# Attention and Fourier mixing of the next batch interleaved with the first MLP of this one, split weights streamed from DRAM

## The chip, the cores and the metric

The kernel runs on one core of a Trainium2 chip. The metric is the device time of one execution in microseconds (us). Engines: PE is TensorE (PEld its weight loads), DVE is VectorE, ACT is ScalarE, POOL is GpSimd, SP is SyncE, which only issues DMAs here.

## The reference

Four batches (B = 4) of 768 tokens, 8 heads of 64, so a width of 512 (DM). Three parts in a row:

```
# windowed attention: per chunk of 32 queries, 8 memory keys and up to 56 neighbours
scores = scale * q_c @ [mem_k, k_ctx].T ;  a = softmax(scores) ;  x = a @ [mem_v, v_ctx]
# Fourier mixing, layer norm, first MLP (512 -> 2048 -> 512)
mixed = real(fft(fft(x, axis=1), axis=2)) ;  u = x + mixed
un = (u - mean) / sqrt(var + 1e-6)
y = u + maximum(un @ w_ch1, 0) @ w_ch2
# gated convolution (512 -> 1024 -> 512)
h = maximum(y @ w_in, 0) ;  conv_out = three taps along the sequence, per channel
out = (h * sigmoid(conv_out)) @ w_out
```

All of it is fp32 in and out.

## The kernel before

Matmuls that need precision are done as three products of fp32r halves: each operand is split into a rounded `_hi` part (a ScalarE copy) and the rest `_lo` (a VectorE or GpSimd subtraction), and `lo*hi + hi*lo + hi*hi` is summed in PSUM. Scores, values and all transposes are plain fp32.

Each engine has a program of its own, written out in order, with semaphores between them. There are three stages.

**Attention and Fourier mixing** (`attention_and_fourier`, line 144 on). A batch has six tiles of 128 tokens (TILES). Per tile: `scores` on TensorE (L490), shift by the maximum and normalisation on VectorE (`softmax`, L388 to L412, with ScalarE's exponential L293 between), `turn` (four transposes, L501) with ScalarE's copy to `p_blk` (L304), `values` (L514) and ScalarE's copy to `x_sb` (L317). Then the Fourier part: the six tiles of x are folded by symmetry (`fold`, L204 to L212; two pairs on GpSimd, one on VectorE), split, multiplied by tables along the sequence (`seq` 0 to 7, nine products each, L525) and along the width (`dim` 0 and 1, 27 products), combined and mirrored (L431 to L446) and transposed back (`mix` 0 to 5, L579). The table ORDER gives for each engine how steps of one batch stand between those of the batch before (a prime behind a step: one batch behind, two primes: two). The buffers of q and k have three tiles (NB), those of v six. x and the mixed tokens are stored to DRAM (`x_scratch`, `mix_scratch`).

**First MLP** (`channel_mlp`), in half batches of 384 tokens. It loads x and the mixed tokens, adds them, normalises, transposes (`turn`, L780) and splits them. All 16 blocks of 128 hidden channels (M1T = 16) of both weights are split once and stay in SBUF. A slot of TensorE is: `expand(m+1)` (twelve products of 384 columns, L791) and `contract(m)` (nine of 512 columns, L806) into three PSUM accumulators (BACC). ScalarE makes `h_hi` (L706), VectorE `h_lo` (L767). At the end of a half, VectorE adds the accumulators to u (L957). 8 halves of 16 slots are 128 slots; the first three expansions and the first two contractions stand at the end of the first stage.

**Gated convolution** (`gated_conv`), which loads y from DRAM (L1039), and the taps (L1049); its weights are loaded and split, and the first batch's y transposed, beside the last half of the MLP (`first_sync`, `first_scalar`, `first_vector`, `first_tensor`). Its first product is L1153.

SyncE's queue issues nearly all DMAs, in order, each behind its waits; the four Fourier tables come from GpSimd's queue.

Of the kernel before, what the change touches and what calls it, by code (L numbers as in the profile page):

```python
# [19 lines left out]
NB = 3  # L20
MIX = 3
# [10 lines left out]
M2T = FF2 // P  # L32
SCALE = float(D) ** -0.5
# [40 lines left out]
class Core:  # L74
# [3 lines left out]
    def __init__(self, nc, ctx, ident):  # L78
# [4 lines left out]
        self.st_x = [self.sem(f"st_x{i}") for i in range(2)]  # L83
        self.st_mix = [self.sem(f"st_mix{i}") for i in range(MIX)]
        self.scored, self.valued, self.x_ready = self.sem("scored"), self.sem("valued"), self.sem("x_ready")
        self.mix_turned, self.mix_ready = self.sem("mix_turned"), self.sem("mix_ready")
        self.st_y = [self.sem(f"st_y{i}") for i in range(2)]
        self.w_ready, self.acc_done, self.y_ready = self.sem("w_ready"), self.sem("acc_done"), self.sem("y_ready")
        self.block = ctx.enter_context(nc.Block())

    def sem(self, name):
# [3 lines left out]
ORDER = {  # L95
    "tensor": (
        "turn5' scores0 seq7'' values5' scores1 "
        "turn0 dim1'' mix0'' mix1'' mix2'' scores2 values0 turn1 seq0' mix3'' values1 seq1' "
        "mix4'' scores3 turn2 seq2' seq3' mix5'' values2 scores4 turn3 seq4' values3 "
        "dim0' scores5 turn4 seq5' values4 seq6'",  # L100
        "turn5' seq7'' values5' dim1'' mix0'' mix1'' mix2'' seq0' mix3'' seq1' mix4'' seq2' mix5'' seq3' mlp3 "
        "seq4' dim0' mlp5 seq5' seq6' mlp7",
        "seq7'' dim1'' mlp9 mix0'' mix1'' mlp10 mix2'' mix3'' mlp11 mix4'' mix5''",
    ),
    "scalar": (
# [13 lines left out]
        "seq6' mlp7",  # L119
        "seq7'' mlp8 dim1'' mlp9 mlp10",  # L120
    ),
}


def attention_steps(engine, attention, starts, ends):

    on = (attention, starts, ends)  # L130
    steps = []
# [1281 lines left out]
```

## Time and profile before

| | |
|---|---|
| timed runs | 1111.16, 1111.59, 1113.31 us; median 1111.59 |
| profiled execution, own time | 1113.53 us |
| its span in the trace | 1111.7 us |
| its mean granted TensorE clock | 0.972 |
| busy in the span | PE 1030.3 us, DVE 494.6, ACT 324.2, POOL 145.2 |
| DMA | 98.75 MB moved, mean 89 GB/s |

The span runs from the first to the last instruction in the trace; start and end of the program lie around it. Busy time of PE counts a matmul until its modelled end, so neighbouring matmuls overlap, and the time of one is read from start to start. The granted clock is given in parts of the upper of TensorE's two levels (1.2 and 2.4 GHz): 1.00 is the upper, 0.50 the lower.

### The profile page before, as it was taken

How to read it: one execution, taken by the hardware profiler on the slowest of the kernel's cores; microseconds unless marked ns; L12 is line 12 of the kernel's file. 1: busy time of each engine (PE TensorE's matmuls, PEld its weight loads, DVE VectorE, ACT ScalarE, POOL GpSimd, SP SyncE). 2: the span in 40 equal slices, each digit the busy share in tenths (PEclk: the TensorE clock that was granted, in tenths of full speed). 3: DMA queues.
4: the chain of work that ended last, by engine and by line, in shares of the span. 5: the costliest groups of instructions: out<-in, count | busy, mean ns of one | idle time of the engine just before them, and what ended most of it. 6: DMA issues, size and time to landing. Idle time of an engine off the chain costs nothing.

```text
span 1111.7 us, 15656 instructions
## 1 busy us (share of the span) xinstructions
PE 1030.3 (93%) x6348; PEld 930.2 (84%) x6348; DVE 494.6 (44%) x749; ACT 324.2 (29%) x551; POOL 145.2 (13%) x97
## 2 busy tenths in 40 slices
PE   5769686968899999999999999999999999999998
PEld 5658676957799989898989898989989798797996
DVE  4466566556453323323222232222439449185390
ACT  3334534445531111111111111111415324243242
POOL 0414141240000000000000000000003204023041
PEclk9889888969999999999999999999999999999999
DMA  9956556153522002020020200105201020110001
GB/s 370 366 190 216 190 193 226 57 170 123 180 86 85 1 1 85 1 85 1 1 85 0 85 0 28 57 1 143 96 29 57 32 83 1 57 57 28 29 1 57
DMA packets 53236, 98.75 MB, mean 89 GB/s; under 512 B 6464, under 2 KB 18880, under 8 KB 52928
## 3 DMA queue, kind: packets, MB, share of 16 engines
q1 hardware_dynamic: 49152, 88.17, 23.0%
q10 hardware_dynamic: 3456, 6.29, 1.5%
q0 software_dynamic: 576, 3.55, 0.8%
q8 instruction: 38, 0.62, 0.2%
q14 instruction: 14, 0.11, 0.0%
HBM read 72.84 MB, written 25.17 MB: 88 GB/s over the span
## 4 chain that ended last, share of the span: by engine, by line
PE 64%; issue 20%; DVE 6%; POOL 6%; DMA 3%; ACT 2%; SPq 0%; ACTq 0%; POOLq 0%; DVEq 0%
PE ps L806 24%; PE ps L791 24%; POOL g_lo L1219 6%; PE ps L525 5%; PE ps L490 3%; PE ps L514 3%; DMA k_nat<-in_k 2%; PE ps L1163 2%; PE ps L579 1%; PE ps L780 1%; PE ps L501 1%; DVE m_all L440 1%; DVE probs L412 1%; DMA y_scratch<-u_sb 0%; DVE stat L406 0%
## 5 line engine op out<-in xcount | busy, mean ns | idle before, releaser
L791 PE MATMUL ps<-un_hi,w 128*128 128x384 f32 x1024 | 284.4, 338 | 2.3 <-ACT mix_sb L350 2.3
L806 PE MATMUL ps<-w,h_hi 128*128 128x512 f32 x768 | 242.0, 396 | 0.0
L767 DVE SCALAR_TENSOR_TENSOR h_lo<-ps,h_hi 128x384 fp32r<-128x384 f32 x128 | 71.3, 557 | 278.7 <-ACT h_hi L706 278.7
L791 PEld LDWEIGHTS ps<-un_hi,w 128*128 128x128 f32 x1024 | 186.6, 188 | 6.7 <-ACT mix_sb L350 2.5
L706 ACT ACTIVATE h_hi<-ps 128x384 fp32r<-128x384 f32 x128 | 63.0, 492 | 374.9 <-PE ps L791 374.5
L791 PE MATMUL ps<-un_lo,w 128*128 128x384 f32 x512 | 171.6, 335 | 0.0
L806 PEld LDWEIGHTS ps<-w,h_hi 128*128 128x128 f32 x768 | 144.3, 188 | 28.3
L806 PE MATMUL ps<-w,h_lo 128*128 128x512 f32 x384 | 151.0, 393 | 0.9 <-DVE h_lo L767 0.9
L1153 PE MATMUL ps<-y_hi,v 128*128 128x384 f32 x512 | 130.6, 334 | 0.8 <-issue 0.8
L1163 PE MATMUL ps<-v,g_hi 128*128 128x512 f32 x384 | 120.5, 395 | 0.0
L1118 DVE SCALAR_TENSOR_TENSOR conv<-h_pad,taps,conv 128x768 f32<-128x768 f32 x64 | 100.4, 1568 | 2.3
L791 PEld LDWEIGHTS ps<-un_lo,w 128*128 128x128 f32 x512 | 96.2, 188 | 4.6
L1219 POOL TENSOR_TENSOR g_lo<-conv,g_hi 128x768 fp32r<-128x768 f32 x32 | 68.6, 2148 | 194.1 <-ACT g_hi L1087 194.1
L1153 PEld LDWEIGHTS ps<-y_hi,v 128*128 128x128 f32 x512 | 92.5, 188 | 1.4 <-issue 1.2
L1163 PEld LDWEIGHTS ps<-v,g_hi 128*128 128x128 f32 x384 | 72.1, 188 | 16.5
L1153 PE MATMUL ps<-y_lo,v 128*128 128x384 f32 x256 | 85.5, 334 | 0.0
L806 PEld LDWEIGHTS ps<-w,h_lo 128*128 128x128 f32 x384 | 72.2, 188 | 13.3 <-DVE h_lo L767 1.2
L1163 PE MATMUL ps<-v,g_lo 128*128 128x512 f32 x192 | 77.5, 404 | 3.8 <-ACT o_sb L1093 3.5
L1213 POOL MEMSET h_pad<- 128x6 f32 x1 | 0.1, 107 | 589.2 <-PE ps L806 589.2
L490 PE MATMUL ps<-k_nat,q_nat 128*64 128x64 f32 x768 | 51.9, 243 | 9.5 <-DMA k_nat<-in_k 9.5
L490 PEld LDWEIGHTS ps<-k_nat,q_nat 128*64 128x64 f32 x768 | 48.5, 154 | 13.0 <-issue 9.9
L525 PE MATMUL ps<-seq_hi,z_lo 128*128 128x386 f32 x96 | 37.9, 394 | 16.4 <-DVE z_lo L417 12.5
(96 smaller groups left out, 1173.3 us busy)
## 6 DMA issues: line engine op xcount, KB each, us to landing
q_nat<-in_q SPq DMA_DIRECT2D x24, 512.0 KB, 4.1
k_nat<-in_k SPq DMA_DIRECT2D x24, 512.0 KB, 5.4
v_win<-in_v SPq DMA_DIRECT2D x24, 512.0 KB, 6.7
w_raw<-in_moe_w_ch SPq DMA_DIRECT2D x32, 256.0 KB, 3.1
x_scratch<-x_sb SPq DMA_DIRECT2D x8, 768.0 KB, 8.2
mix_scratch<-mix_sb ACTq DMA_DIRECT2D x24, 256.0 KB, 2.1
u_sb<-x_scratch SPq DMA_DIRECT2D x8, 768.0 KB, 4.6
mix_in<-mix_scratch SPq DMA_DIRECT2D x8, 768.0 KB, 6.2
```

The source lines that it names most:

```text
L412: nc.vector.tensor_tensor(probs[:, t % 2], e, total.unsqueeze(2).to_broadcast([P, H, KEYS]), ALU.mult).then_inc(p_ready, 1)
L490: last = nc.tensor.matmul(ps[64 * y:64 * y + 64, BS[t % 2], (2 * a + x) * KEYS:(2 * a + x + 1) * KEYS], q_blk[:, t % NB, a, c].rearrange(" ...
L514: last = nc.tensor.matmul(ps[64 * y:64 * y + 64, BO, h * D:(h + 1) * D], p_blk[:, t % 2, 4 * a + 2 * y + u].rearrange("p x j -> p (x j)"), ...
L525: last = nc.tensor.matmul(out, lhs, rhs, start=(n == 0), stop=(n == 3 * len(terms) - 1))
L706: nc.scalar.activation(h_hi[:, m % 2, :], ps[:, BH + m % 2, 0:HALF], ACT.Relu).then_inc(h_hi_ready, 1)
L767: nc.vector.scalar_tensor_tensor(out=h_lo[:, m % 2, :], in0=ps[:, BH + m % 2, 0:HALF], scalar=0.0, in1=h_hi[:, m % 2, :].bitcast(F32), op0 ...
L791: last = nc.tensor.matmul(ps[:, BH + m % 2, 0:HALF], w[:, cols], x[:, par, c, :], start=(k == 0), stop=(k == 3 * ND - 1))
L806: last = nc.tensor.matmul(ps[:, BACC[s], :], h[:, m % 2, cols], w, start=(m == 0 and j == 0), stop=(m == M1T - 1 and j == 2))
L1118: nc.vector.scalar_tensor_tensor(out=c, in0=h[:, j:S + j], scalar=taps[:, m, j:j + 1], in1=c, op0=ALU.mult, op1=ALU.add).then_inc(tap_done ...
L1153: last = nc.tensor.matmul(ps[:, BH[m % 2] + half, 0:HALF], w[:, cols], y[:, c, toks], start=(k == 0), stop=(k == 3 * ND - 1))
L1163: last = nc.tensor.matmul(ps[:, BACC[t % 3], :], g[:, m, cols], w, start=(m == 0 and j == 0), stop=(m == M2T - 1 and j == 2))
L1219: nc.gpsimd.tensor_tensor(g_lo[:, m, :], conv[:, m % 3, :], g_hi[:, m, :].bitcast(F32), ALU.subtract).then_inc(g_lo_ready, 1)
```

## The change

The first two stages become one function, `mixing_and_mlp`. Batch 0 goes through attention, mixing and normalising alone (PROLOGUE). Then come 128 slots (B x SLOTS, 32 for a batch); in each, TensorE issues `expand(n+1)`, then the words that DURING has for this slot, for the batch after, then `contract(n)`. The other engines do the same with their words behind `hidden(n+1)`. All loops are written out.

- x isn't stored: `mix` is added to it in SBUF (`add_mix`, one function on VectorE with three additions per tile in place of ScalarE's three copies to `mix_sb`), and y is made in the same buffer. `x_scratch` and `mix_scratch` are gone.
- SBUF has only three blocks of split weights (NW). During the first half of batch 0 the raw weights are loaded and split (slots 1 to 13: `weights`), and each split block is stored to `w_scratch`; from slot 13 on each block is loaded from there again for each half batch, 0.5 MB for each of the two weights per slot.
- q, k and v have two buffers each (NB = 2).
- At the end of a half, VectorE's additions (`finish`) stand behind `hidden(n+1)`.

```diff
-NB = 3
+NB = 2
+NW = 3
+NRAW = 2
+PROLOGUE = {
+    "tensor": "scores0 scores1 turn0 scores2 values0 turn1 scores3 values1 turn2 scores4 values2 turn3 scores5 "
+              "values3 turn4 values4 turn5 values5 seq0 seq1 seq2 seq3 seq4 seq5 seq6 seq7 dim0 dim1 "
+              "mix0 mix1 mix2 mix3 mix4 mix5 un0 un1 un2",
...
+DURING = {
     "tensor": (
+        "un3'", "un4' scores0", "un5'", "scores1 turn0", "values0", "scores2 turn1", "values1", "scores3 turn2",
...
+            for n in range(B * SLOTS):
+                b, s = divmod(n, SLOTS)
+                if b + 1 < B:
+                    if s in (2, 4, 6, 8):
+                        load_tile(b + 1, s // 2 + 1)
+                    if s in (5, 7, 9, 11):
+                        load_values(b + 1, s // 2)
...
+                if 3 <= n + 2 < M1T:
+                    store_split(n + 2)
+                    if n + 2 + NRAW < M1T:
+                        load_raw(n + 2 + NRAW)
+                if M1T <= n + 3 < B * SLOTS:
+                    load_split(0, n + 3)
+                if M1T <= n + 2 < B * SLOTS:
+                    load_split(1, n + 2)
+                if s == M1T + 1:
+                    store_y(b, 0)
...
+                if n >= (2 * B - 1) * M1T:
+                    conv_sync(sp, n - (2 * B - 1) * M1T)
...
+            def load_split(which, n):
+                if which == 0:
+                    sp.wait_ge(h_done, n - NW + 1)
+                else:
+                    sp.wait_ge(contracted, n - NW + 1)
...
+                sp.dma_start(w_all[n % NW][:, which].bitcast(F32), w_dram[which, n % M1T]
+                             ).then_inc((ld_w1, ld_w2)[which][n % NW], 16)
...
+            run(0, PROLOGUE["vector"])
+            hidden(0)
+            for n in range(B * SLOTS):
...
+                if n + 1 < B * SLOTS:
+                    hidden(n + 1)
+                if s in (0, M1T) and n > 0:
+                    finish(n - 1)
+                words = DURING["vector"][s]
...
+            expand(0)
+            for n in range(B * SLOTS):
+                b, s = divmod(n, SLOTS)
+                if n + 1 < B * SLOTS:
+                    expand(n + 1)
+                words = DURING["tensor"][s]
+                run(b + 1, words if b + 1 < B else " ".join(w for w in words.split() if w.endswith("'")))
+                contract(n)
+                if n >= (2 * B - 1) * M1T:
+                    conv_tensor(pe, n - (2 * B - 1) * M1T)
```

`contract(n)` waits, as before, for the additions of the half before where m is 0 (`y_ready`). The convolution's loads are now spread over the slots of the last half (`first_sync(sp, k)`; k = 1 is slot 113).

TensorE, in the attention of batch 1. Before, values, scores and the transposes of probabilities (L514, L490, L501) stand between products of the sequence transform of batch 0:

```order
L525 MATMUL ps<-seq_hi,z_lo 128x386
L525 MATMUL ps<-seq_lo,z_hi 128x386
L525 MATMUL ps<-seq_hi,z_hi 128x386
L514 MATMUL ps<-v_win,p_blk 64x64 x16
L490 MATMUL ps<-k_nat,q_nat 64x64 x16
L501 MATMUL ps<-ident_sb,probs 128x128 x4
L525 MATMUL ps<-seq_hi,z_lo 128x386
```

After the change a values step (L724) stands between the end of an expansion (L814) and a contraction (L832) of batch 0:

```order
L814 MATMUL ps<-un_hi,w_63 128x384 x2
L814 MATMUL ps<-un_lo,w_63 128x384
L814 MATMUL ps<-un_hi,w_63 128x384
L724 MATMUL ps<-v_win,p_blk 64x64 x16
L832 MATMUL ps<-w_62,h_lo 128x512
L832 MATMUL ps<-w_62,h_hi 128x512 x2
```

Attention of batch 1 has moved from the Fourier products of batch 0 into the MLP of batch 0.

VectorE, where a half batch ends. Before, the three additions (L957) stand directly behind `h_lo` of the half's last block, and ahead of the next half's first:

```order
L761 TENSOR_TENSOR un_lo<-ps,un_hi 128x4x128
L767 SCALAR_TENSOR_TENSOR h_lo<-ps,h_hi 128x384
L957 TENSOR_TENSOR u_sb<-ps,u_sb 128x512 x3
L962 UNCONDITIONAL_BRANCH
L962 ISA
L767 SCALAR_TENSOR_TENSOR h_lo<-ps,h_hi 128x384
```

After (L611 is `h_lo`, L236 to L244 the fold of batch 1, L625 the additions, `xu_51` the tokens of batch 0):

```order
L611 SCALAR_TENSOR_TENSOR h_lo<-ps,h_hi 128x384 x3
L236 TENSOR_TENSOR z_raw<-xu_52 128x512
L237 TENSOR_TENSOR z_raw<-xu_52 128x512
L240 TENSOR_TENSOR dve_half<-z_raw 128x512
L241 TENSOR_TENSOR z_raw<-z_raw 128x2x256
L243 TENSOR_TENSOR z_raw<-dve_half 128x2x128
L244 TENSOR_TENSOR z_raw<-dve_half 128x2x128
L611 SCALAR_TENSOR_TENSOR h_lo<-ps,h_hi 128x384
L625 TENSOR_TENSOR xu_51<-ps,xu_51 128x512 x3
L515 TENSOR_TENSOR z_lo<-z_raw,z_hi 128x1024
```

The `h_lo` ahead of the additions belongs to the second block of the next half (n+1), whose expansion is issued before the contraction that waits for the additions.

SyncE, in the last half. Before, the queue stands there with a y store, the y load, the taps and the raw weights of the convolution:

```order
L888 DMA y_scratch<-u_sb 128x3x512
L1039 DMA y_in<-y_scratch 128x6x512
L1049 DMA taps<-in_moe_conv_w 128x8x1 x3
L1057 DMA v_raw<-in_moe_w_in 128x4x128
L1059 DMA v_raw<-in_moe_w_out 128x512
```

After, in slots 112 to 114 (`w_61` to `w_63` are the three weight buffers):

```order
L294 DMA w_61<-w_scratch 128x1024
L294 DMA w_63<-w_scratch 128x1024
L294 DMA w_62<-w_scratch 128x1024
L299 DMA y_scratch<-xu_52 128x3x512
L908 DMA y_in<-y_scratch 128x6x512
L918 DMA taps<-in_moe_conv_w 128x8x1 x3
L924 DMA v_raw<-in_moe_w_in 128x4x128
L927 DMA v_raw<-in_moe_w_out 128x512
L294 DMA w_61<-w_scratch 128x1024
L294 DMA w_63<-w_scratch 128x1024
```

The streamed weights of slots 116 and 117 now stand behind the taps on the same queue.

## Rows read from the trace of the kernel before

**Rows 1.** Three stages by windows; columns: window, length, busy and count per engine, clock.
```profile
0.00:288.30 288.30, 215.93 (x2190) 198.27 (x2190) 164.30 (x280) 123.00 (x232) 76.49 (x64) 0.89 0.60 211
288.30:827.10 538.80, 537.04 (x2743) 484.04 (x2743) 171.30 (x323) 98.43 (x180) 0.11 (x1) 1.00 0.15 48
827.10:1111.70 284.60, 277.30 (x1416) 247.87 (x1416) 159.05 (x146) 102.75 (x139) 68.56 (x32) 1.00 0.12 42
```

**Rows 2.** Chain that ended last: start, duration, what, in the MLP.
```profile
321.12 2.10 PE ps L806 x9
325.74 2.10 PE ps L806 x9
329.92 2.10 PE ps L806 x9
```

**Rows 3.** TensorE timeline, attention between Fourier products; start, duration, line, operation.
```profile
74.30 0.34 PE L525 MATMUL ps<-seq_lo,z_hi 128*128 128x386 f32 x1
74.48 0.33 PE L525 MATMUL ps<-seq_hi,z_hi 128*128 128x386 f32 x1
74.74 1.90 PE L490 MATMUL ps<-k_nat,q_nat 128*64 128x64 f32 x32
...
77.25 0.34 PE L525 MATMUL ps<-seq_lo,z_hi 128*128 128x386 f32 x1
...
85.83 1.90 PE L514 MATMUL ps<-v_win,p_blk 128*64 128x64 f32 x32
...
87.94 0.34 PE L525 MATMUL ps<-b_lo,dim_hi 128*128 128x386 f32 x1
```

**Rows 4.** Timeline of a steady MLP slot around an expansion's end.
```profile
402.57 0.39 PE L806 MATMUL ps<-w,h_lo 128*128 128x512 f32 x1
...
403.77 0.54 DVE L755 TENSOR_SCALAR un<-u_sb,mv,root 128x512 f32<-128x512 f32 x1
```

**Rows 5.** Groups by line, 230 to 830 us: busy, mean ns, idle before.
```profile
L957 DVE TENSOR_TENSOR u_sb<-ps,u_sb 128x512 f32<-128x512 f32 x24 | 16.6, 692 | 28.4 <-PE ps L806 28.3
```

**Rows 6.** TensorE timeline where the second network's expansion begins.
```profile
827.06 0.41 PE L1153 MATMUL ps<-y_hi,v 128*128 128x384 f32 x1 [0.83 <-issue]
```

**Rows 7.** Timeline of VectorE, first tile of batch 0.
```profile
10.09 0.69 DVE L388 TENSOR_REDUCE stat<-ps 128x8 f32<-128x512 f32 x1 [7.07 <-PE ps L490]
...
13.68 0.69 DVE L412 TENSOR_TENSOR probs<-probs,stat 128x512 f32<-128x512 f32 x1
```

**Rows 8.** TensorE timeline, scores behind a wait for their load.
```profile
30.33 2.77 PE L490 MATMUL ps<-k_nat,q_nat 128*64 128x64 f32 x32 [2.26 <-DMA k_nat<-in_k]
```

**Rows 9.** DMA issues in 130 to 170 us: count, KB each, median us to landing.
```profile
v_win<-in_v SPq DMA_DIRECT2D x4, 512.0 KB, 5.6
```

**Rows 10.** Windows: DMA rates, two VectorE chains, one fold on GpSimd.
```profile
16.00:18.00 2.00, 2.00 (x47) 2.00 (x44) 0.93 (x3) 0.94 (x2) 0.00 (x0) 1.00 1.10 427
292.50:298.50 6.00, 6.00 (x32) 5.32 (x31) 3.66 (x6) 1.44 (x2) 0.00 (x0) 1.00 0.78 249
761.00:775.00 14.00, 14.00 (x71) 12.51 (x70) 2.23 (x4) 1.90 (x4) 0.00 (x0) 1.00 0.96 264
...
38.05:45.10 7.05, 3.78 (x54) 3.40 (x52) 4.33 (x7) 2.41 (x4) 6.84 (x6) 0.97 1.03 410
250.10:254.00 3.90, 3.12 (x20) 2.57 (x19) 3.59 (x14) 2.99 (x6) 0.00 (x0) 1.00 0.18 67
261.60:264.00 2.40, 2.40 (x15) 2.40 (x14) 2.30 (x7) 1.80 (x3) 0.00 (x0) 1.00 0.00 0
```

**Rows 11.** Timeline between batch 0's attention and its first Fourier product.
```profile
56.38 5.10 POOL L272 TENSOR_TENSOR z_lo<-z_raw,z_hi 128x1024 fp32r<-128x1024 f32 x2 [4.62 <-ACT z_hi L324]
56.56 2.72 DVE L412 TENSOR_TENSOR probs<-probs,stat 128x512 f32<-128x512 f32 x1
...
67.36 0.66 PE L525 MATMUL ps<-seq_hi,z_lo 128*128 128x386 f32 x1 [7.37 <-DVE z_lo L417]
```

**Rows 12.** SyncE's queue, issue of the convolution taps.
```profile
760.54 7.81 SPq L1049 DMA_DIRECT2D taps<-in_moe_conv_w  x3
```

More of the change, by code:

```diff
@@ L32 @@
 M2T = FF2 // P
+SLOTS = 2 * M1T
 SCALE = float(D) ** -0.5
@@ L133, in attention_steps, with steps, mixing_and_mlp @@
+def steps(words):
+    out = []
+    for word in words.split():
         step = word.rstrip("'")
         name = step.rstrip("0123456789")
-        steps.append((name, int(step[len(name):]), len(word) - len(step)))
-    return [step for step in steps if on[step[2]] or step[0] == "mlp"]
-def attention_and_fourier(core, q, k, v, seq_tab, dim_tab, x_dram, mix_dram):
+        out.append((name, int(step[len(name):]), len(word) - len(step)))
+    return out
+def mixing_and_mlp(core, ins, w_dram, y_dram):
@@ L353, in turn, with square_root, upper @@
-            def turn(b, attention, starts, ends):
-                for step, t, behind in attention_steps("scalar", attention, starts, ends):
+                nc.scalar.activation(q_sin[:, ab, :], ps[:, DIM_BANKS[ab][1], 0:NF], ACT.Copy).then_inc(sin_kept, 1)
+            def square_root(b, half):
+                g = 2 * b + half
+                act.wait_ge(var_done, g + 1)
+                nc.scalar.activation(root[:, half, 1, :], root[:, half, 0, :], ACT.Sqrt).then_inc(root_done, 1)
+            def upper(b, s):
+                act.wait_ge(un_turned, b * TILES + s + 1)
+                nc.scalar.activation(un_hi[:, s // SUBS, :, s % SUBS * P:(s % SUBS + 1) * P],
+                                     ps[:, un_bank(b, s), :].rearrange("p (c n) -> p c n", c=ND), ACT.Copy
+                                     ).then_inc(un_hi_ready, 1)
@@ new lines, in finish @@
+            def finish(n):
+                b, half = n // SLOTS, n % SLOTS // M1T
+                g = 2 * b + half
+                for s in range(SUBS):
+                    if s < SUBS - 1:
+                        dve.wait_ge(acc_done, g * (SUBS - 1) + s + 1)
+                    else:
+                        dve.wait_ge(contracted, n + 1)
+                    y = xu[b % 2][:, half * SUBS + s, 0:DM]
+                    nc.vector.tensor_tensor(y, ps[:, ACC[s], :], y, ALU.add).then_inc(y_ready, 1)
@@ L458, in turn, with run @@
+            def run(b, words):
+                for step, t, behind in steps(words):
+                    at = b - behind
+                    if step == "scores":
                         shift(at, t)
@@ L578, in turn_mix, with turn_un @@
                         j = 2 * mm + ab
-                        last = nc.tensor.transpose(ps[:, bank("mix", t), j * P:(j + 1) * P],
+                        last = nc.tensor.transpose(ps[:, RING[t % 3], j * P:(j + 1) * P],
                                                    m_all[:, mm, ab, t * P:(t + 1) * P], ident_sb[:])
                 last.then_inc(mix_turned, 1)
-            def turn(b, attention, starts, ends):
-                for step, t, behind in attention_steps("tensor", attention, starts, ends):
+            def turn_un(b, s):
+                n = b * TILES + s
+                pe.wait_ge(un_ready, n + 1)
+                if b > 0 and s < SUBS:
+                    pe.wait_ge(u_ready, n + 4)
+                elif b > 0:
+                    pe.wait_ge(un_lo_ready, n - 2)
+                for c in range(ND):
+                    last = nc.tensor.transpose(ps[:, un_bank(b, s), c * P:(c + 1) * P], un[:, s % 2, c * P:(c + 1) * P],
+                                               ident_sb[:])
+                last.then_inc(un_turned, 1)
@@ L585, in turn, with run @@
+            def run(b, words):
+                for step, t, behind in steps(words):
                     at = b - behind
-                    if step == "mlp":
-                        mlp_tensor(pe, t)
-                    elif step == "scores":
+                    if step == "scores":
                         scores(at, t)
```

886 lines of the change are left out of this document (352 added, 534 removed), and 25 rows, old and new, of tables (DURING, ORDER, PROLOGUE).

## The prediction

> **What bounds it now.** I read the busy windows first, cut where the work changes. Between 0 and 288.3 us (attention and Fourier mixing of four batches, and the first two MLP slots) TensorE is busy 215.9 us, so it idles 72.4 us, and its granted clock averages 0.89. Between 288.3 and 827.1 us it is busy 537.0 of 538.8 us at clock 1.00; the gated convolution behind it takes 284.6 us [rows 1]. So the MLP stage is a solid row of matmuls, and only the first stage has something to give: idle time and time at the low clock. The chain view gives the price of the solid row: one MLP slot (expand a block of 128 hidden channels, contract the one before) takes 4.18 us, and 4.62 us where four transposes stand in it, so these cost 0.44 [rows 2]. 128 slots make 535.0 us in either kernel.
>
> The convolution stage keeps its code, so the question is when its first matmul starts: at 827.06 us now, 1.0 us behind the last contraction (0.83 of it idle) [rows 6]. I price the new kernel to that point. Everything is set against the profiled execution: span 1111.70, own time 1113.53; the median of the timed runs is 1111.59, so a difference in the span carries over to the median as it is.
>
> **The solid part after the change.** Attention and mixing of batches 1 to 3 stand between an expansion and a contraction. They are no cheaper in TensorE time, only covered by it. The nearest rows are attention steps between Fourier products at the full clock [rows 3]. From the product at 74.48 to the one at 77.25, less two normal steps of 0.175 (74.30 to 74.48): scores and one transpose of probabilities cost 2.42 us. Values: 85.83 to 87.94, less 0.175, plus the 0.085 gap that stands ahead of such a group (74.48+0.175 to 74.74): 2.02. A batch has six values (12.1), five scores with a transpose (12.1), and one scores and one transpose apart (2.4): 26.6. Fourier: 99 products (72 along the sequence, 27 along the width) at 0.175 are 17.4, six mixing transposes at 0.44 are 2.6. Together 46.6, for three batches 139.7 us. Further 21 transposes of normalised tokens and 6 of the convolution's tokens, 27 at 0.44: 11.9. With the handover of 1.0: 535.0 + 139.7 + 11.9 + 1.0 = 687.6 us. From below this holds to 1 or 2 us (the rows are back to back at the clock's upper level); the additional waits on weight semaphores have no row, 0 to 0.04 us each on 112 slots, taken as 0, up to 4.
>
> **New waits at half-tile boundaries.** VectorE's order changes there: before, the three additions of the finished half stand ahead of the next block's `h_lo`; after, `h_lo` of block n+1 stands first, then the additions (`finish`). The first contraction of a half waits for the additions. So it can't start when its expansion ends: an expansion ends at 402.57, VectorE is through with `h_lo` at 403.77 [rows 4], the first addition takes 0.69 [rows 5], with the wake-up 1.95 us. Queued behind that wait on TensorE is everything else; ScalarE and VectorE wait for TensorE in turn. At slot 16 nothing covers it (four times 1.95), at slot 0 a transpose covers 0.44 (three times 1.5): 12.3 us. The cover that hides `fold2` on VectorE (3.4 us in slot 15) is just long enough; if it overruns by 0.7 that is 2 us in all.
>
> **The prologue.** Batch 0 now has nothing beside it, and its q, k and v buffers shrink to two, v from six. Tile t+1's q and k are issued behind v of tile t, which waits for values of tile t-2. I step through it. The first scores end at 10.0, VectorE starts at 10.09 and is through with one tile at 14.37, that is 4.3 with the exponential inside [rows 7]; now a second tile's scores and shift stand first, so values 0 end near 20 (an estimate that hardly counts, as the loads decide next). Before tile 3's q and k are there, the Fourier tables (3.55 MB) and v of tile 2 must pass: 5.1 MB from about 14.4 us on, at 410 to 427 GB/s [rows 10], end near 27.2. From there a loop: scores 2.8 us at the lower clock level (2.77 where they stood behind a wait of 2.26; 1.90 at the upper) [rows 8, 3], values the same 32 passes, 2.8, then v, q, k from issue to landing 6.7 us (v issued third lands 5.6 after its own issue, 1.05 after q's) [rows 9]. Tile 4's loads stand behind two pairs of raw weights, 1.05 MB at 249/0.78 = 319 GB/s, 3.3 us [rows 10]. So values 1 end at 27.2 + 5.6 = 32.8, values 2 at 32.8 + 6.7 + 3.3 + 5.6 = 48.4, values 3 at 48.4 + 12.3 = 60.7, and tile 3 of x is there at 61.3.
>
> GpSimd then folds two pairs, 7.0 us each by its first (six operations) [rows 10], and 6.6 for the second, and makes two `z_lo`, 5.1 [rows 11]: done at 80.0. Before, the first Fourier product started 5.9 us after those two (61.48 to 67.36) [rows 11], because VectorE's fold and split trail them. Now VectorE is free earlier: bounds 80.0 and 85.9, taken 84.0, nearer to the row. The Trainium skill, SBUF — State Buffer, section "Who interferes with whom", says that a VectorE tensor_tensor with two SBUF inputs fully blocks against a GpSimd operation that reads SBUF; the row agrees (2.72 us beside the `z_lo`, against 0.69 alone), and a fold blocked at each operation would give the upper bound, 1.9 us later.
>
> Then in series: 99 products 17.4; 2.6 for a start at the lower clock (67.36 also started there); twice ScalarE's copy and VectorE's combination and one mirror, 4.1 (combine and mirror together lie inside a 2.4 us window); three mixing transposes and their additions 3.3; statistics, root and Newton step 3.8; nine VectorE operations of normalising, adding and splitting 6.3 [rows 10]. Sum 37.5: the MLP's first expansion stands at 121.5. It starts at the lower clock, and two expansions lose 2.6 us.
>
> **Streams.** The split weights need 1.05 MB per slot, 251 GB/s where nothing else runs; with q, k, v of a tile per two slots (12.8 us) it is 3.67 MB, 287 GB/s, under the 415. Each load is issued about 2.5 slots, over 10 us, ahead. Two places are tighter. In slots 2 to 11 of batch 0 the weights are still being split: two slots store 2.1 MB, load 1.05 MB raw and 1.57 MB q, k, v. At 415 and 319 GB/s that is 12.1 us against 12.8, and some 4 us of slack in the order: 0, but see below. In slot 113, SyncE issues a y store, the y load and the taps, whose issue holds it for 7.81 us [rows 12], ahead of the weights for slots 116 and 117; now these transfers harmed nobody. From the start of slot 113 (DMA begins at 2.0), these pass: one weight load (1.35); the y store, y load and taps (8.5: the 14 us window at 0.96 share held them and three raw pairs of 1.65) [rows 10]; a raw pair (1.65); the weight load itself (1.35). That is 14.85, and with about 1 us to completion 15.9; expansion 117 wants it at 3 x 4.18 + 0.44 = 13.0. So 2.9 us, bounds 0 and 7.
>
> **Sum.** 121.5 + 2.6 + 687.6 + 12.3 + 2.9 = 826.9, against 827.06 now. What three batches' idle time gives back is paid for by an uncovered prologue and the new waits. Forecast: no change, 1112 us (rounded). A measurement of this kernel can tell about 0.2%, 2.2 us.
>
> **Rivals.**
> 1. Faster. The loop of loads and the clock are both kinder: scores and values at the upper level save 1.9 us a loop, three times 5.7; the fold unblocked saves 4.0; no stall at the taps 2.9. All would be 1099; two of the three about 1102. For it: the clock was 1.00 in 16 to 18 us [rows 10]. Against: here the idle in each loop is about 6.7 us, and 2.26 was enough [rows 8].
> 2. Slower, by DMA in batch 0's first half. It decides where the rate falls under 4.72 MB / 12.8 us = 369 GB/s. With stores and 512-byte reads mixed in at 290, two slots take 16.3, so three pairs cost 10.5: 1122. For it: this mix has no row, and raw weights alone reach only 319. Against: 410 beside a store of x [rows 10]. The Trainium skill, DMA: Bandwidth & Descriptors, Specifications, gives about 358 GB/s as HBM's limit per core; no row here shows it (427 was reached), and by it the two slots take 13.2, which the slack would swallow: 1112 still, but near the edge.
> 3. Slower, by the prologue: if each of the three landings takes 1.2 us more than the 6.7 of [rows 9], and each of the six strided mixing additions, which have no row, 1.5 us instead of my 0.9, it ends 7 us later; with the fold at its upper bound 9: 1120. It decides from 2.2 us on. For it: the loop has three landings in series and nothing beside them.
>
> **How the numbers follow.** Forecast 0.38 (1106 to 1117; of it 0.12 faster than the bound, 0.16 within, 0.10 slower), rival 1 0.30, rival 2 0.18, rival 3 0.14. Faster 0.42, same 0.16, slower 0.42. The range 1100 to 1124 leaves out the ends of rivals 1 and 2, and takes in the bounds of fold, taps and semaphores. The likeliest case's own range is 1106 to 1117.
>
> **What would show it.** First expansion at 121.5 (rival 1: under 115, rival 3: 128 or more). Slots of 6.6 and 6.2 us in turn with attention in them, 4.18 without. TensorE waits named by the addition on VectorE: four of 1.9, three of 1.5. One wait for a weight load of about 3 us some 45 us before the convolution, none in batch 0 (rival 2: several there, on TensorE or behind ScalarE's weight copies). First product of the convolution within 5 us of 827, and 284.6 us after it. The prediction is wrong if attention steps cost more between MLP matmuls than 2.42 and 2.02, as then three batches multiply the error, or if the streams are late in every batch.

## The result, and the profile after

The changed kernel takes 1128.22 us (median; 1126.98 to 1131.2), the kernel before 1112.45 us (1111.16 to 1115.02) on the same chip. The ratio is 1.0143, 95% interval 1.0114 to 1.0172: slower, where the forecast was no change, and above the forecast's range. The profiled execution has a span of 1129.4 us at a mean granted clock of 0.962.

First the busy windows, cut at the first expansion and at the convolution stage's first product (window, length, busy time and count of TensorE, its weight loads, VectorE, ScalarE and GpSimd, granted clock, DMA share and rate):

```profile
0.00:129.70 129.70, 65.81 (x543) 60.09 (x544) 55.97 (x104) 29.90 (x46) 21.75 (x24) 0.75 0.47 170
129.70:844.05 714.35, 697.23 (x4390) 632.15 (x4390) 274.67 (x548) 174.78 (x300) 57.03 (x43) 0.99 0.69 244
844.05:1129.40 285.35, 277.71 (x1416) 248.10 (x1416) 159.63 (x146) 102.63 (x139) 69.33 (x32) 1.00 0.12 42
```

The convolution stage is what it was (285.35 against 284.60 us) [rows 1]. It begins at 844.05 us, 17.0 us later than before and 17.2 later than the forecast's 826.9. Of that, 8.2 us lie ahead of the first expansion (129.70 against 121.5 forecast) and 8.95 behind it (714.35 against 826.9 - 121.5 = 705.4). The middle stretch isn't idle much: 17 us of 714. But its clock is 0.99, not the 1.00 of [rows 1].

TensorE's waits over the whole program (what was waited for: us in total, times, longest):

```profile
PE ps L692 <- DMA k_win<-in_k: 23.7, 5, 7.8
PE ps L832 <- DVE xu L625: 11.7, 7, 1.9
PE ps L735 <- DVE z_lo L515: 11.3, 1, 11.3
PE ps L708 <- DVE probs L510: 8.9, 5, 3.6
PE ps L795 <- DVE un L593: 4.6, 2, 3.6
PE ps L814 <- DMA w<-w_scratch: 4.6, 1, 4.6
PE ps L735 <- DVE b_lo L521: 3.9, 1, 3.9
```

The second row is the forecast's waits at the half-tile boundaries: four of 1.86, three of 1.42, 11.7 us against 12.3 forecast. The row of 4.6 is the one at the taps (2.9 forecast). The last one, 3.9, isn't in the forecast at all. Here it is on the timeline of all engines (SPq is SyncE's queue; start, duration, engine, line, operation, idle before and what ended it):

```profile
93.61 0.81 SPq L281 DMA_DIRECT2D w_scratch<-w  x2
...
94.46 0.72 SPq L273 DMA_DIRECT2D raw<-in_moe_w_ch  x1
...
95.23 1.28 SPq L276 DMA_DIRECT2D raw<-in_moe_w_ch  x1
...
101.02 1.06 ACT L435 ACTIVATE w<-raw 128x1024 fp32r<-128x1024 f32 x1 [4.41 <-DMA raw<-in_moe_w_ch]
...
103.12 0.69 PE L735 MATMUL ps<-b_hi,dim_lo 128*128 128x386 f32 x1 [3.93 <-DVE b_lo L521]
```

ScalarE's copy of weights 2 (L435) stands ahead of its copies of the last two sequence blocks. The raw weights it reads go into a buffer that is free only when weights 0 are split, so SyncE issues them at 94.46, and they are there at 101. VectorE's `b_lo` and TensorE's width products stand behind. When they start, a product takes 0.69 us (the first) at the lower clock.

Behind a boundary of batch 2, on TensorE:

```profile
607.76 0.34 PE L814 MATMUL ps<-un_hi,w 128*128 128x384 f32 x1
609.96 0.47 PE L832 MATMUL ps<-w,h_lo 128*128 128x512 f32 x1 [1.86 <-DVE xu L625]
610.27 1.01 PE L832 MATMUL ps<-w,h_hi 128*128 128x512 f32 x2
611.08 0.63 PE L832 MATMUL ps<-w,h_lo 128*128 128x512 f32 x1
```

A contraction product with `h_lo` that took 0.39 us ahead of the wait (605.17) takes 0.63 us behind it (611.08). The contraction that starts here lasts 3.68 us (609.96 to 613.64) against 2.16 where it stands behind a wait and nothing falls. The same happens at 233.45 and 421.69, not at 771.55. So the wait costs more than its own length. The three together lose 4.73 us: contractions of 2.79, 3.22 and 3.68 us in place of 2.16, expansions behind them of 3.01, 2.61 and 2.17 in place of 2.09. The granted clock is 0.71 in each of the three stretches from the contraction to the end of that expansion, and 1.00 in the 4 us behind the wait at 771.55.

At the taps, in SyncE's queue and on TensorE:

```profile
774.26 0.43 SPq L299 DMA_DIRECT2D y_scratch<-xu  x1
774.81 0.42 SPq L908 DMA_DIRECT2D y_in<-y_scratch  x1
775.27 8.70 SPq L918 DMA_DIRECT2D taps<-in_moe_conv_w  x3
784.01 0.58 SPq L924 DMA_DIRECT2D v_raw<-in_moe_w_in  x1
...
791.38 0.69 PE L814 MATMUL ps<-un_hi,w 128*128 128x384 f32 x1 [4.58 <-DMA w<-w_scratch]
```

The issue of the taps holds SyncE 8.70 us (7.81 before) [rows 12], and the expansion behind the wait takes 3.67 us, 1.57 more than its 2.10.

### The profile page after: what moved, and what is told of

Same layout as the page of the kernel before. It is cut to its first block, busy times and chain, and to the rows that moved or that the text cites. A ratio compares the mean times of both kernels' runs of the same rounds, so it can differ in the third digit from the quotient of the medians.

```text
span 1129.4 us, 15243 instructions
## 1 busy us (share of the span) xinstructions
PE 1040.7 (92%) x6348; PEld 940.3 (83%) x6348; DVE 490.3 (43%) x797; ACT 307.3 (27%) x485; POOL 148.1 (13%) x99
## 4 chain that ended last, share of the span: by engine, by line
PE 66%; issue 17%; POOL 6%; DMA 4%; DVE 3%; SPq 2%; ACT 1%; POOLq 0%
PE ps L814 24%; PE ps L832 24%; PE ps L735 6%; POOL g_lo L1087 6%; PE ps L692 4%; PE ps L724 4%; DMA k_win<-in_k 2%; PE ps L1031 2%; PE ps L708 1%; PE ps L795 1%; SPq L918 1%; PE ps L782 1%; DVE xu L625 1%; DMA w<-w_scratch 1%; DMA raw<-in_moe_w_ch 1%
## 5 line engine op out<-in xcount | busy, mean ns | idle before, releaser
L814 PE MATMUL ps<-un_hi,w 128*128 128x384 f32 x1024 | 287.0, 341 | 7.0 <-DMA w<-w_scratch 4.6
L832 PE MATMUL ps<-w,h_hi 128*128 128x512 f32 x768 | 242.2, 397 | 0.0
L611 DVE SCALAR_TENSOR_TENSOR h_lo<-ps,h_hi 128x384 fp32r<-128x384 f32 x128 | 71.4, 558 | 355.3 <-ACT h_hi L439 355.1
L814 PEld LDWEIGHTS ps<-un_hi,w 128*128 128x128 f32 x1024 | 191.5, 192 | 12.6 <-DMA w<-w_scratch 4.8
L814 PE MATMUL ps<-un_lo,w 128*128 128x384 f32 x512 | 174.6, 341 | 0.0
L832 PEld LDWEIGHTS ps<-w,h_hi 128*128 128x128 f32 x768 | 146.0, 190 | 27.9
L832 PE MATMUL ps<-w,h_lo 128*128 128x512 f32 x384 | 158.4, 412 | 11.7 <-DVE xu L625 11.7
L814 PEld LDWEIGHTS ps<-un_lo,w 128*128 128x128 f32 x512 | 98.2, 192 | 5.5
L832 PEld LDWEIGHTS ps<-w,h_lo 128*128 128x128 f32 x384 | 72.6, 189 | 26.1 <-DVE h_lo L611 13.5
L236 POOL TENSOR_TENSOR z_raw<-xu 128x512 f32<-128x512 f32 x8 | 12.2, 1531 | 505.5 <-ACT xu L398 505.4
L692 PE MATMUL ps<-k_win,q_blk 128*64 128x64 f32 x768 | 52.6, 244 | 23.7 <-DMA k_win<-in_k 23.7
L692 PEld LDWEIGHTS ps<-k_win,q_blk 128*64 128x64 f32 x768 | 49.1, 156 | 29.0 <-DMA k_win<-in_k 18.3
L724 PEld LDWEIGHTS ps<-v_win,p_blk 128*64 128x64 f32 x768 | 46.7, 149 | 9.9 <-issue 9.9
```

The costliest lines, as they stand in the source:

```text
L236: api.tensor_tensor(z_raw[:, i, 0, :], xa, xb, ALU.add).then_inc(added, 1)
L611: nc.vector.scalar_tensor_tensor(out=h_lo[:, n % 2, :], in0=ps[:, BH[n % 2], 0:HALF], scalar=0.0, in1=h_hi[:, n % 2, :].bitcast(F32), op0= ...
L692: last = nc.tensor.matmul(ps[64 * y:64 * y + 64, scores_bank(b, t), (2 * a + x) * KEYS:(2 * a + x + 1) * KEYS], q_blk[:, t % NB, a, c].rea ...
L724: last = nc.tensor.matmul(ps[64 * y:64 * y + 64, RING[2], h * D:(h + 1) * D], p_blk[:, t % 2, 4 * a + 2 * y + u].rearrange("p x j -> p (x ...
L814: last = nc.tensor.matmul(ps[:, BH[n % 2], 0:HALF], w[:, cols], x[:, half, c, :], start=(j == 0), stop=(j == 3 * ND - 1))
L832: last = nc.tensor.matmul(ps[:, ACC[s], :], h[:, n % 2, cols], w, start=(m == 0 and j == 0), stop=(m == M1T - 1 and j == 2))
```

## Experiments

All edits are to the changed kernel. Its time is 1128.22 us, and a measurement tells about 2 us. Two positions in each trace divide an effect: the first expansion (129.70 us in the changed kernel) and the convolution's first product (844.05), with 714.35 us between them.

**Drain first.** VectorE adds the finished half to the tokens before it makes the next `h_lo`.

```
+                if s in (0, M1T) and n > 0:
+                    finish(n - 1)
                 if n + 1 < B * SLOTS:
                     hidden(n + 1)
-                if s in (0, M1T) and n > 0:
-                    finish(n - 1)
```

> VectorE's three additions at the end of a half stand ahead of the next h_lo again; nothing else changes. Theory A (the additions make TensorE wait, and the low clock seen for some 4 us behind three of these waits is a consequence of the wait): the waits of 4 x 1.86 and 3 x 1.42 = 11.7 us go, and so do the slow matmuls behind the waits of batches 0 to 2, 4.6 us together; the convolution's first product comes at 827.7 instead of 844.05, the time falls by 16.3 us. Rival B (the low clock comes from the thinner attention work in the slots ahead, and would fall anyway): 11.7 us only. Rival C (another semaphore ends the wait nearly as late): under 5 us.

Measured: 1119.73 us (1118.68 to 1121.65), ratio to before 1.0062 (1.0044 to 1.0079); first expansion at 132.42, first convolution product at 834.47, so 702.05 us between them: 12.3 less. TensorE's waits over the whole program:

```profile
PE ps L814 <- DMA w<-w_scratch: 6.2, 1, 6.2
...
PE ps L832 <- DVE xu L625: 3.1, 3, 1.0
```

And its timeline at the boundary of batch 2 that was shown above:

```profile
603.01 0.47 PE L832 MATMUL ps<-w,h_lo 128*128 128x512 f32 x1 [1.04 <-DVE xu L625]
603.33 0.63 PE L832 MATMUL ps<-w,h_hi 128*128 128x512 f32 x2
603.79 0.39 PE L832 MATMUL ps<-w,h_lo 128*128 128x512 f32 x1
```

At the same place the wait is 1.04 instead of 1.86 us, only the first product behind it reads longer, and the clock doesn't fall. The 12.3 us can be placed from start to start of the products. Three waits are 0.82 shorter and four are gone, which moves the products behind them by 9.49 us (three of the latter by 1.67 each, one by 2.02, since idle time counts only from the modelled end of the product ahead). The 4.73 us of low clock went too. The first two expansions took 6.47 us in place of 7.08, as their low clock ended sooner. At the taps 2.56 us came back: a wait of 6.18, an expansion of 4.00 and a contraction of 2.73 in place of 4.58, 3.67 and 2.10. That makes 12.27, with differences of up to 0.5 us either way that nearly cancel. So the 12.3 us, near to rival B's 11.7 by number, don't speak for it; the timelines do, and they show theory A. Neither of the two sums on record allowed for the three waits of 1.04 that stay or for the taps.

The two profiled executions differ by 9.6 us and the medians by 8.5, as the prologue, which the edit doesn't touch, was 2.7 us longer in this one (its waits for keys sum to 26.1 us against 23.7).

**Weights 2 late.** ScalarE and VectorE split weights 2 at the end of the prologue.

```
-              "weights1 seq4 seq5 weights2 seq6 seq7 dim0 dim1 root0 un0 un1 un2 root1",
+              "weights1 seq4 seq5 seq6 seq7 dim0 dim1 root0 un0 un1 un2 root1 weights2",
...
-              "softmax5 fold2 split2 seq0 seq1 seq2 weights0 seq3 seq4 weights1 seq5 seq6 weights2 seq7 "
...
+              "softmax5 fold2 split2 seq0 seq1 seq2 weights0 seq3 seq4 weights1 seq5 seq6 seq7 "
...
```

> In the prologue, the split of the third weight block (weights2) moves from between seq6 and seq7 to the very end on ScalarE and VectorE. Theory A (this split's wait for its raw load blocks ScalarE in front of the sequence products' copies, TensorE idles 3.9 us and runs the next 15 products at the lower clock): the first expansion comes 6 us earlier, at 123.6 instead of 129.7, and the whole falls by 5 to 6 us. Rival B (the idle time would be taken up by another link, or the clock falls anyway at the next wait, for the copy of the sine part): 0 to 3 us.

Measured: 1124.53 us (1122.35 to 1125.6), ratio 1.0101 (1.0083 to 1.0119). The first Fourier product starts at 85.04 (84.91 in the changed kernel), the first expansion at 123.68 in place of 129.70; between these two 38.64 us in place of 44.79. The stretch behind stays (714.79). So the wait and the low clock that it brings cost 6.1 us, nearly all in the Fourier products (23.66 against 29.80 us from the first product to the first mixing transpose). The median fell by 3.7 us, less than the 5 to 6 expected; the two profiled executions differ by 5.6.

**Taps at the end.** SyncE issues the taps 13 slots later, in slot 126 instead of 113.

```
             load(sp, 0)
+        if k == 14:
             with nc.allow_non_contiguous_dma(reason="three taps per channel, once"):
```

> The three DMAs of the convolution taps are issued in slot 126, behind the last streamed weights, instead of in slot 113 in front of those of slots 116 and 117. Theory A (the taps, whose issue held SyncE 8.7 us, make the weights late): the wait of 4.58 us and the slow expansion behind it (1.6) go, 6 us less in all, and the convolution doesn't wait for the taps at its start. Rival B (the 2.4 MB of y store and y load in front are what makes them late): a wait of 1 to 4 us stays, the gain is under 3 us. Rival C: the taps are late for the first convolution, and the gain is lost there.

Measured: 1123.05 us (1121.78 to 1128.08), ratio 1.0103 (1.0071 to 1.0135). Of TensorE's wait for a weight load 0.34 us is left; first expansion at 128.99, first convolution product at 836.91, 707.92 us between them: 6.4 less. Of that, the wait is 4.24 (4.58 less 0.34), the expansion behind it 1.47 (3.67 to 2.20), and the first two expansions, 6.40 us in place of 7.08, are 0.7, which the edit doesn't touch. The low clock came behind three of the four waits of 1.86 here too, but one of them is another: not the one at 608.47, but the one at 768.19.

**Values first.** In the prologue TensorE makes the values of tile t before the scores of tile t+2.

```
-    "tensor": "scores0 scores1 turn0 scores2 values0 turn1 scores3 values1 turn2 scores4 values2 turn3 scores5 "
-              "values3 turn4 values4 turn5 values5 seq0 seq1 seq2 seq3 seq4 seq5 seq6 seq7 dim0 dim1 "
+    "tensor": "scores0 scores1 turn0 values0 scores2 turn1 values1 scores3 turn2 values2 scores4 turn3 values3 "
+              "scores5 turn4 values4 turn5 values5 seq0 seq1 seq2 seq3 seq4 seq5 seq6 seq7 dim0 dim1 "
```

> In the prologue's TensorE order, values of tile t stand ahead of scores of tile t+2 instead of behind them, so that the loads that wait for values are issued earlier; buffers stay at two. Theory A (the loop values, load, scores in series makes the prologue long): waits for k fall from 23.7 us to under 8, tile 3 of x comes some 10 us earlier, and the first Fourier product 7 us earlier (from there GpSimd's folds decide), 78 instead of 84.9; the time falls by 6 to 8 us. Rival B (GpSimd's folds and the blocked VectorE fold decide the start of the Fourier part whatever the loads do): under 2 us.

Measured: 1129.04 us (1126.68 to 1130.4), ratio 1.0142 (1.0121 to 1.0164): no gain. The trace says why:

```profile
PE ps L708 <- DVE probs L510: 16.5, 5, 3.5
...
PE ps L692 <- DMA k_win<-in_k: 6.8, 2, 6.4
```

The waits for keys fell from 23.7 to 6.8 us, but those for the shares rose from 8.9 to 16.5. VectorE's order wasn't changed: it shifts the scores of tile t+2 before it normalises tile t+1. So the values of tile t, the scores and shift of tile t+2 and the shares and transposes of tile t+1 now stand in series, 11 us a tile (transposes at 15.39, 26.61, 37.61 and 48.30). On VectorE:

```profile
23.38 0.69 DVE L485 TENSOR_REDUCE stat<-ps 128x8 f32<-128x512 f32 x1 [8.04 <-PE ps L692]
24.10 0.69 DVE L490 TENSOR_TENSOR probs<-ps,stat 128x512 f32<-128x512 f32 x1
24.71 0.68 DVE L504 TENSOR_REDUCE stat<-probs 128x8 f32<-128x512 f32 x1
...
25.86 0.69 DVE L510 TENSOR_TENSOR probs<-probs,stat 128x512 f32<-128x512 f32 x1
```

The first Fourier product came at 82.07 and the first expansion at 127.56, 2.8 and 2.1 us earlier than in the changed kernel. Five executions with the old order have their first Fourier product at 84.91 to 87.95, so a small gain may be real; the median doesn't show it.

**The three repairs together** (drain first, weights 2 late, taps at the end).

> The three repairs at once: the drain of the accumulators ahead of the lower half on VectorE, the split of weights 2 at the end of the prologue, the taps at the program's end. By the theory that each took away a stall of its own, the stretches add up: first expansion near 123.7 us (as with weights 2 alone), the stretch from there to the first convolution product 714.35 - 12.3 - 6.4 = 695.6 us, so that product at 819.3 us, 24.7 us ahead of the changed kernel's 844.05, and a time near 1103.5 us, ratio to the kernel before 0.992. By the rival that the three share a cause (the TensorE clock falls somewhere in any case, and a stall removed comes back as low clock), the medians of the single runs add at best: 1128.2 - 8.5 - 3.7 - 5.2 = 1110.8 us or more, no difference from before.

Measured: 1105.3 us (1104.88 to 1108.06), ratio 0.9938 (0.9924 to 0.9953): faster than the kernel before. First expansion at 124.56, first convolution product at 818.04 (819.3 expected). So the three are separate stalls. Between the two points lie 693.48 us, 2.1 less than the 695.6 of the expectation: the 2.6 us that came back at the taps with drain first alone don't come back here.

**Keys ahead.** Only the order of SyncE's first loads.

```
-            for t in range(TILES):
-                load_tile(0, t)
-                load_values(0, t)
-                if t == 3:
-                    load_raw(0)
-                    load_raw(1)
+            for word in "k0 v0 k1 v1 k2 k3 k4 v2 k5 v3 raw0 raw1 v4 v5".split():
+                {"k": load_tile, "v": load_values, "r": lambda _, m: load_raw(m)}[word[0]](0, int(word[-1]))
```

> Only the order of SyncE's first loads is changed: the keys of tiles 3, 4 and 5 are issued ahead of the values of tiles 2, 3 and 4. Theory: the prologue's waits for keys (23.7 us, 5 times) come from the queue's order, since the keys of tile t+1 stand behind the values of tile t, whose wait ends only with values t-2. Then the waits behind the first fall from 17.4 us to under 5, the last attention output is copied near 58 us in place of 73.7, the first expansion starts 12 to 18 us earlier (112 to 118 us), and the time is 1110 to 1116 us. Rival: the transfers themselves are the limit (the core's DMA moved over 400 GB/s in this stretch), so the values come late in place of the keys; the first expansion moves by under 4 us and the time stays above 1124 us.

Measured: 1108.86 us (1106.94 to 1112.8), ratio 0.9970 (0.9954 to 0.9986). The first expansion is at 109.93, 19.8 us earlier, above what was expected. Here is SyncE's queue in the changed kernel: the values of tile 2 at 21.39, and directly behind them q and keys of tile 3:

```profile
9.62 0.33 SPq L259 DMA_DIRECT2D q_blk<-in_q  x1
9.99 0.43 SPq L260 DMA_DIRECT2D k_win<-in_k  x1
21.39 0.33 SPq L267 DMA_DIRECT2D v_win<-in_v  x1
21.76 0.43 SPq L259 DMA_DIRECT2D q_blk<-in_q  x1
```

And with keys ahead, where those of tile 3 go at 12.92, as soon as the second scores have freed their buffer:

```profile
9.61 0.33 SPq L259 DMA_DIRECT2D q_blk<-in_q  x1
9.98 0.43 SPq L260 DMA_DIRECT2D k_win<-in_k  x1
12.92 0.33 SPq L259 DMA_DIRECT2D q_blk<-in_q  x1
...
23.14 0.33 SPq L267 DMA_DIRECT2D v_win<-in_v  x1
```

The loop of loads that the forecast stepped through was no limit of the transfers. It came of a queue in which a load that has to wait (values, two buffers) stands ahead of one that could go (keys). With six value buffers the kernel before had no wait for a value buffer in front of its keys in batch 0.

**Splits on VectorE.** In the first batch VectorE makes the lower parts of all three folded pairs.

```
+                if b == 0:
+                    pool.wait_ge(pool_lo_ready, 2)
+                else:
                     for i in range(2):
                         lower(b, i)
...
-                                        ).then_inc(dve_lo_ready, 1)
+                                        ).then_inc(dve_lo_ready if i == 2 else pool_lo_ready, 1)
...
-              "softmax5 fold2 split2 seq0 seq1 ...
+              "softmax5 split0 fold2 split1 split2 seq0 seq1 ...
```

> Only in the first batch, VectorE makes the lower parts of the first two folded pairs (1.2 us each) in place of GpSimd (2.8 us each, from 75.54 to 81.07 us, beside VectorE's fold whose two middle additions took 2.72 and 2.82 us where the same form took 0.69 us alone). Theory (the two engines hold each other up): VectorE's fold takes 4 us in place of 8.2, TensorE's wait for the last lower part falls from 11.3 to about 8 us, first expansion 2.5 to 4 us earlier, time near 1125 us. Rival (the additions are slow for another reason, or VectorE's two extra subtractions fill the gain): within 1 us of the changed kernel, 1128 us.

Measured: 1127.15 us (1125.35 to 1129.02), ratio 1.0132 (1.0112 to 1.0151): by the time alone, nothing. The changed kernel's VectorE, with GpSimd at its splits (75.54 to 81.07):

```profile
74.91 1.21 DVE L237 TENSOR_TENSOR z_raw<-xu 128x512 f32<-128x512 f32 x1
76.16 2.72 DVE L240 TENSOR_TENSOR dve_half<-z_raw 128x512 f32<-128x512 f32 x1
78.80 2.82 DVE L241 TENSOR_TENSOR z_raw<-z_raw 128x512 f32<-128x512 f32 x1
```

With the splits on VectorE, where GpSimd is through with its second fold at 79.20:

```profile
77.42 1.21 DVE L237 TENSOR_TENSOR z_raw<-xu 128x512 f32<-128x512 f32 x1
78.66 1.09 DVE L240 TENSOR_TENSOR dve_half<-z_raw 128x512 f32<-128x512 f32 x1
79.67 0.68 DVE L241 TENSOR_TENSOR z_raw<-z_raw 128x512 f32<-128x512 f32 x1
```

The same two operations take 1.77 in place of 5.54 us, and from the last attention output's copy to the first Fourier product it is 7.5 us (76.13 to 83.64) in place of 11.2 (73.67 to 84.91). The mechanism holds; its 3.7 us were there, but the loads ahead landed 2.5 us later in this execution, and the first expansion moved by 1.6. Whether the median moves is inconclusive.

**All five.**

> All five edits together. If they are separate stalls, the time is that of the three repairs less what keys ahead and the splits on VectorE give alone: 1103.5 - 14 - 3 = 1086 us, ratio to before 0.977. If the prologue meets another limit (the table loads, 3.5 MB from the 16th us on, or the raw weights, all in the same first 60 us), half of that: 1095 us.

Measured: 1080.69 us (1079.03 to 1081.92), ratio 0.9709 (0.9695 to 0.9724), below both expectations. First expansion at 101.47 (129.70 less 6.1, 19.8 and 1.6 is 102.2), then 693.47 us, as with three repairs. A wait of 1.26 us for streamed weights stands in that stretch (0.16 with three repairs), though the taps are issued late; it is 1.50 and 1.94 us in the two kernels below. Why it grew is not shown. The expectation was too high because it took 14 us for the keys.

**Shares first** and **split behind**, two more steps in the prologue. The first lets VectorE make the shares of tile t+1 before it shifts the scores of tile t+2; the second, on top, moves ScalarE's split of the first folded pair behind the last tile's copies, and VectorE's lower part of that pair behind its own fold.

```
-    "vector": "scores0 scores1 softmax0 scores2 softmax1 scores3 softmax2 scores4 softmax3 scores5 softmax4 "
+    "vector": "scores0 scores1 softmax0 softmax1 scores2 softmax2 scores3 softmax3 scores4 softmax4 scores5 "
```
```
-              "softmax5 values3 turn4 values4 split0 turn5 values5 split1 split2 seq0 ...
+              "softmax5 values3 turn4 values4 turn5 values5 split0 split1 split2 seq0 ...
...
-              "softmax5 split0 fold2 split1 split2 seq0 ...
+              "softmax5 fold2 split0 split1 split2 seq0 ...
```

> The kernel of all five edits, and in the prologue VectorE makes the shares of tile t+1 before it shifts the scores of tile t+2 (they were behind it). Theory: a tile's 5.8 us there is the loop scores 1.9, shift 1.4, normalisation 2.5, transposes; with the shares off that loop, TensorE's own work (scores, transposes, values: 4.3 us) sets the pace, the four inner tiles take 1.5 us less each, the first expansion starts near 96 us in place of 101.5, and the time is 1076 us. Rival: ScalarE's split of the first folded pair, which stands ahead of the last transposed shares and waits for GpSimd's fold (48.2 us), and GpSimd's two folds of 6.8 us behind tile 3 hold the end of the prologue; then the first expansion moves by 2 to 4 us.

Measured: 1078.18 us (1077.05 to 1080.51), ratio 0.9686 (0.9665 to 0.9707). The first expansion is at 99.49, 2.0 us earlier, at the lower edge of what the rival allowed. Its windows, to be read against the three at the top:

```profile
0.00:99.49 99.49, 59.60 (x543) 54.74 (x544) 54.46 (x105) 28.73 (x45) 17.66 (x22) 0.79 0.56 206
99.49:793.31 693.82, 688.36 (x4390) 625.30 (x4390) 275.84 (x549) 175.64 (x301) 56.96 (x43) 1.00 0.74 253
793.31:1078.70 285.39, 277.74 (x1416) 248.12 (x1416) 159.66 (x146) 102.64 (x139) 69.33 (x32) 1.00 0.12 42
```

The pace of the inner tiles did rise (the copies of the second to fifth attention output stand at 25.29, 35.14, 39.66 and 44.71 in place of 27.76, 35.58, 41.33 and 47.62), but a wait for keys of 4.14 us (0.62 before) took a part of it, and at the last values TensorE waited for ScalarE's copy behind that split, 4.09 us in place of 3.24:

```profile
49.47 3.28 PE L723 MATMUL ps<-v_win,p_blk 128*64 128x64 f32 x32 [4.09 <-ACT p_blk L387]
```

> As the run before, and ScalarE's split of the first folded pair stands behind the last tile's copies, so that the last values needn't wait for GpSimd's fold (3.2 us of TensorE's time with five edits). Theory: the last attention output comes 3 to 4 us earlier, but TensorE's Fourier products then wait for GpSimd's second fold; the first expansion gains 1.5 to 3 us on the run before. Rival: the second fold alone sets the start of the Fourier products, gain under 0.7 us.

Measured: 1078.77 us (1078.35 to 1080.77), ratio 0.9695 (0.9673 to 0.9716). The last values start at 46.46 in place of 49.47, and the wait moves to the Fourier products (from 7.5 to 11.0 us):

```profile
59.35 0.66 PE L734 MATMUL ps<-seq_hi,z_lo 128*128 128x386 f32 x1 [11.03 <-DVE z_lo L514]
```

The first expansion gains 0.6 us, as the rival's number said. Its cause is shown only in part. GpSimd's two folds stand one after the other from 40.09 to 55.19 us, but VectorE's own fold stands beside the second one and ends later, and its three lower parts stand behind that:

```profile
49.00 1.14 DVE L236 TENSOR_TENSOR z_raw<-xu 128x512 f32<-128x512 f32 x1 [5.88 <-ACT xu L397]
50.06 1.74 DVE L237 TENSOR_TENSOR z_raw<-xu 128x512 f32<-128x512 f32 x1
51.84 1.63 DVE L240 TENSOR_TENSOR dve_half<-z_raw 128x512 f32<-128x512 f32 x1
53.40 1.21 DVE L241 TENSOR_TENSOR z_raw<-z_raw 128x512 f32<-128x512 f32 x1
...
55.72 3.48 DVE L514 TENSOR_TENSOR z_lo<-z_raw,z_hi 128x1024 fp32r<-128x1024 f32 x3
```

Which of the two folds sets this point, no run tells apart.

## Why the forecast was wrong

Most of the miss comes from three stalls: a queued split that the prologue's chain left out, low clock behind waits that were costed at their length alone, and taps that held weight loads up longer than the forecast said. Step by step, the two points of the trace give the account: 17.2 us late in all.

**Up to the first Fourier product: right.** 84.91 us against 84.0. The term rests on landings that scatter (this product stands at 84.91 to 87.95 in five executions with the same code up to it), so it is in part luck that it came this close. What the step missed is that its loop was a choice of the queue's order, worth 19.8 us, as keys ahead shows. The forecast had named that order and priced it, but took it as given.

**Failed step 1: "Then in series ... Sum 37.5".** It measured 44.79 (84.91 to 129.70). I summed copies and combinations of that chain, and left out what else stands in the queues of the same engines: weights 2 on ScalarE between sequence blocks 5 and 6, whose raw load can only be issued behind the split of weights 0. With the split moved away, the same chain takes 38.64, 1.1 above the term. This failure cost 6.15 us.

**Failed step 2: the boundaries "12.3".** The waits themselves are right: 1.86 and 1.42 against 1.95 and 1.5, 11.7 in all. What failed is that a wait was costed as its own length. The clock fell behind three of the four waits of 1.86 and took 4.73 us more. Over the six executions that have these waits (the changed kernel; weights 2 late, taps at the end, values first, keys ahead, splits on VectorE), the clock fell behind 16 of 24 waits of 1.86 us and behind none of 18 of 1.42. Over the five that drain first it fell behind none of 15 of 1.04, at places where the longer wait had brought it down.

**Taps "2.9": the mechanism right, the size off.** The wait measured 4.58 and the slow expansion behind it 1.57, together 6.15, inside the term's bounds of 0 and 7. Again the part left out is the clock, and the issue held SyncE 0.9 us longer than in [rows 12].

**The solid part "687.6": right.** In the run with shares first, 693.82 us lie between the two points. Less three waits of 1.04, the wait of 1.50 for streamed weights, and the first expansion with its neighbour at 5.82 us (4.18 at the full clock), that is 687.6, the term itself. The changed kernel gives 714.35 - 11.7 - 4.73 - 6.15 - (7.08 - 4.18) = 688.87, 1.3 us above it. That rest goes with the seven boundary waits: from the transposes at 323.34 to the contraction behind the wait it is 2.02 us, where drain first, without a wait, has 0.35, so a wait listed as 1.42 costs 1.67; the four of 1.86 cost 0.16 more than listed. Attention between MLP products costs what the rows from between Fourier products said.

**Rivals.** Slower by DMA in batch 0's first half: not so, TensorE waited for no weight load there. Faster by a kinder loop and clock: not so. Slower by the prologue came nearest in size (128 or more was its mark, 129.70 measured), but by another mechanism than its landings: the chain behind the first Fourier product.

The sum of what failed: 0.9 (first Fourier product) + 6.15 + 1.15 (rest of the chain), the 8.2; and 4.73 (low clock behind the boundaries) + 3.25 (taps) + 1.3 (the boundary waits beyond their listed length) + 0.3 (first expansions, 2.9 against 2.6) - 0.6 (waits, 11.7 against 12.3), the 8.95. The wait for weights 2, the low clock behind the boundaries, 8.6 of the 11.7 us of boundary waits and the stall at the taps go away without touching the change's idea. With the keys ahead in their queue as well, and the two smaller steps in the prologue, the same idea gives 3.1%: 1078.18 against 1112.77 us.

## What to carry to other kernels

When a chain is priced, walk the whole queue of every engine in it, also the steps of other work that stand between its links, and ask of each when its input could be issued at all. A wait in a nearly solid row of matmuls costs its length and may cost the slower products behind it too: look in the trace for a wait of the same size, and read what followed it. A gain near the sum on record isn't yet its cause: drain first came out near the wrong theory's number, and only the products behind the wait told the two apart. When a buffer count is cut, the load that now waits is the smaller part of it; what is queued behind that load is the larger, and an order by readiness may give it back for nothing (19.8 us here).

## What I had not expected of the hardware

The granted clock fell from its upper level (2.4 GHz) to the lower (1.2 GHz) in a stretch where TensorE had been busy back to back for tens of microseconds, behind an idle time as short as 1.86 us, in 16 of 24 cases; behind 1.42 and 1.04 us of idle at like places in none of 33. Drain first shows it for one and the same place (1.86 and 1.04 us); the waits of 1.42 stand at others. What decides between the 16 and the 8 stays open: no run here tells it apart. A wait for streamed weights of 1.94 us, in the run with split behind, had no fall behind it either (granted clock 1.00 in the 4 us after it).

VectorE's additions of 128x512 took 2.72 and 2.82 us beside GpSimd's subtraction of 128x1024, 1.09 and 0.68 when that was taken away. The Trainium skill, SBUF — State Buffer, section "Who interferes with whom", says that such operations of the two engines block each other; the trace agrees: 2.72 us, where the fold's first operation, ahead of that subtraction, took 0.69.

The issue of three small transfers, the taps, held SyncE's queue for 8.70 us (7.81 before), while the issue of the load of half a megabyte of weights ahead of them at 773.90 held it for 0.32.
